# Moving 20 on-chip buffers to other addresses and taking out one small write on GpSimd

## The reference

```python
# attention: B=2, H=8 heads, S=768, D=64, 16 clusters a head
q_assign = argmax(q_n @ c_n.T); k_assign = argmax(k_n @ c_n.T)
mask   = q_assign[..., :, None] == k_assign[..., None, :]
scores = where(mask, scale * q @ k.T, -1e9)
x      = softmax(scores) @ v                      # -> (1536, 512)
# mixture of 8 experts, each row goes to one
e      = argmax(x @ w_gate);  gate = softmax(x @ w_gate)[e]
x      = gate * (relu(x @ w1[e]) @ w2[e])         # w1: 512x1024, w2: 1024x512
# last layer, hidden width 1536
out    = ((x @ w_a) * (x @ w_b)) @ w_out
```

## Time and profile before

| | before |
|---|---|
| median of 3 runs | 809.38 us |
| lowest, highest | 809.35, 809.58 us |
| the profiled execution's own time | 809.58 us |
| its span in the trace | 807.8 us |
| PE busy | 797.6 us (99%) |
| PEld busy | 678.3 us (84%) |
| DVE busy | 459.1 us (57%) |
| ACT busy | 359.0 us (44%) |
| POOL busy | 365.2 us (45%) |

### The profile page before, as it was taken

The page is one execution under the profiler, slowest core; times in us unless marked ns, Lnnn a source line. Parts: engine busy times, 40 slices in busy tenths (PEclk is TensorE's granted clock), DMA queues, the critical chain, the costliest instruction groups (busy, mean ns, idle before and its releaser), DMA issues.

```text
span 807.8 us, 13176 instructions
## 1 busy us (share of the span) xinstructions
PE 797.6 (99%) x4412; PEld 678.3 (84%) x4413; DVE 459.1 (57%) x716; ACT 359.0 (44%) x740; POOL 365.2 (45%) x311
## 2 busy tenths in 40 slices
PE   8999999999999999999999999999999999999997
PEld 5899999999998688888888888888888888888886
DVE  5987988988997989999867004531211112121211
ACT  7877867877786443443434444111212112121112
POOL 6798898888982354464454634000311002010001
PEclk9999999999999999999999999999999999999999
DMA  7463363363242487888677313300101000010001
GB/s 202 115 190 95 105 185 94 102 187 95 63 125 84 152 255 201 250 251 253 220 212 235 113 41 99 123 1 14 27 14 53 1 14 13 1 53 0 1 1 52
DMA packets 48665, 86.62 MB, mean 107 GB/s; under 512 B 17856, under 2 KB 19904, under 8 KB 48624
## 3 DMA queue, kind: packets, MB, share of 16 engines
q1 hardware_dynamic: 41888, 69.36, 29.9%
q0 software_dynamic: 3856, 11.33, 4.9%
q10 hardware_dynamic: 2880, 5.39, 1.8%
HBM read 73.29 MB, written 11.30 MB: 105 GB/s over the span
## 4 chain that ended last, share of the span: by engine, by line
PE 77%; issue 16%; DVE 2%; DMA 2%; POOL 1%; ACT 1%; SPq 0%; POOLq 0%; DVEq 0%
PE bank L1729 9%; PE bank L1659 9%; PE bank L1463 7%; PE bank L1626 7%; PE bank L1628 7%; PE bank L1627 7%; PE bank L1666 4%; PE bank L1733 4%; PE bank L1432 4%; PE bank L1477 4%; PE bank L1453 4%; PE bank L1479 3%; PE bank L1501 2%; PE bank L1391 2%; PE bank L1673 2%
## 5 line engine op out<-in xcount | busy, mean ns | idle before, releaser
L1355 DVE TENSOR_TENSOR ab_raw<-bank,a_sb 128x512 f32<-128x512 f32 x35 | 24.2, 692 | 183.9 <-PE bank L1628 183.9
L409 DVE CAST w_split<-stage 128x1024 fp32r<-128x1024 f32 x68 | 70.0, 1029 | 68.2 <-PE bank L1666 52.7
L1128 DVE TENSOR_REDUCE neg_max<-bank 128x1 f32<-128x768 f32 x96 | 91.6, 955 | 23.4 <-PE bank L1453 22.5
L846 ACT ACTIVATE pT_hi<-bank 128x384 fp32r<-128x384 f32 x192 | 83.9, 490 | 43.0 <-PE bank L1463 42.4
L413 DVE TENSOR_TENSOR w_split<-stage,w_split 128x1024 fp32r<-128x1024 f32 x72 | 99.3, 1382 | 2.4
L1096 DVE TENSOR_TENSOR pT_lo<-bank,pT_hi 128x384 fp32r<-128x384 f32 x192 | 97.5, 550 | 2.2 <-ACT pT_hi L846 1.7
L717 POOL TENSOR_TENSOR hT_lo<-hT_raw,hT_hi 128x512 fp32r<-128x512 f32 x38 | 54.6, 1437 | 78.0 <-ACT hT_raw L921 77.9
L866 ACT ACTIVATE probs<-bank,neg_max 128x768 f32<-128x768 f32 x96 | 87.1, 907 | 3.4 <-DVE neg_max L1128 3.2
L1729 PE MATMUL bank<-w_split,hT_hi 128*128 (+1 forms) x304 | 79.5, 404 | 0.0
L981 ACT ACTIVATE a_sb<-bank 128x512 f32<-128x512 f32 x35 | 20.9, 597 | 131.9 <-PE bank L1628 131.9
L1463 PE MATMUL bank<-ident,probs 128*128 128x128 f32 x576 | 78.9, 273 | 0.1
(11 more groups left out here) (269 smaller groups left out, 1735.9 us busy)
## 6 DMA issues: line engine op xcount, KB each, us to landing
stage<-w SPq DMA_DIRECT2D x64, 512.0 KB, 4.5
q_raw<-qT SPq DMA_DIRECT2D x32, 192.0 KB, 3.7
k_raw<-kT SPq DMA_DIRECT2D x32, 192.0 KB, 4.0
sorted_y<-y_sb ACTq DMA_DIRECT2D x19, 257.0 KB, 4.7
q_pair<-qT SPq DMA_DIRECT2D x8, 384.0 KB, 4.7
v_raw<-v_keys SPq DMA_DIRECT2D x16, 192.0 KB, 4.1
stage<-w_a SPq DMA_DIRECT2D x6, 512.0 KB, 4.6
stage<-w_b SPq DMA_DIRECT2D x6, 512.0 KB, 4.9
```

The costliest lines, as they stand in the source:

```text
L1128: dve.tensor_reduce(neg_max[:, qt % 2:qt % 2 + 1], scores[qt % 2][:, 0:S], AX_X, ALU.max, negate=True).then_inc(s_max, 1)
```

## The change

Two things change, in one edit. First, buffers are declared in another order, and three fillers change in size: `gap_to_x_in` (480 bytes) goes, `last_scope_room` shrinks by 480 bytes, `past_attention` by 3,392. Nothing else about the buffers changes, neither shape nor type. Second, the write at L704 goes, and with it the second increment of `s_spare_i`.

```diff
--- before.py
+++ after.py
@@ -61,16 +61,16 @@
             return ctx.enter_context(nc.semaphore(name))
 
 
-        tri = sb("tri", [P, P], BF16)
-        token_tile = sb("token_tile", [P, T, 1], F32)
         ident = sb("ident", [P, P], F32)
         ident_bf = sb("ident_bf", [P, P], BF16)
         factors = sb("factors", [P, 2], F32)
+        tri = sb("tri", [P, P], BF16)
         ones = sb("ones", [P, P], BF16)
         e_minus = sb("e_minus", [P, T, E], F32)
         row_no = sb("row_no", [P, 1, P], BF16)
         row_no1 = sb("row_no1", [P, 1, P], BF16)
         tile_row = sb("tile_row", [P, 1, TILES], F32)
+        token_tile = sb("token_tile", [P, T, 1], F32)
         token_lane = sb("token_lane", [P, 1], F32)
         slot_row = sb("slot_row", [P, T], I32)
         slot_tile = sb("slot_tile", [P, T], F32)
@@ -100,6 +100,7 @@
         e_start_i = sb("e_start_i", [P, E], I32)
         first_pair = sb("first_pair", [P, T, 2], BF16)
         e_zero = sb("e_zero", [P, T // 2], BF16)
+        spare_i = sb("spare_i", [P, 1], I32)
         first_f = sb("first_f", [P, 1], F32)
         first_i = sb("first_i", [P, 1], I32)
         gate2 = sb("gate2", [P, T], F32)
@@ -122,9 +123,15 @@
 
         att = ExitStack()
         sb("first_expert_weights", [P, HELD, 2, CH], F32R, att)
+        c_minus = sb("c_minus", [P, C], F32, att)
         cen_rows = sb("cen_rows", [P, 2, D], F32, att)
+        exp_spare = sb("exp_spare", [P, 1], F32, att)
+        cen_sq = sb("cen_sq", [P, D], F32, att)
+        cen_n = sb("cen_n", [P, 8], F32, att)
         cen_pair = sb("cen_pair", [P, PAIRS, 2, C], F32, att)
+        mask_line = sb("mask_line", [P, 2], F32, att)
         back_w = sb("back_w", [P, G, XW], F32, att)
+        gate_w = sb("gate_w", [P, H, E], F32, att)
         q_pair = sb("q_pair", [P, S], F32, att)
         k_pair = sb("k_pair", [P, S], F32, att)
         q_raw = sb("q_raw", [P, 2, S], F32, att)
@@ -138,11 +145,6 @@
         hot_rows = sb("hot_rows", [P, S], F32, att)
         probs = sb("probs", [P, 2, S], F32, att)
         o_T = sb("o_T", [P, HALF], F32, att)
-        c_minus = sb("c_minus", [P, C], F32, att)
-        cen_sq = sb("cen_sq", [P, D], F32, att)
-        cen_n = sb("cen_n", [P, 8], F32, att)
-        mask_line = sb("mask_line", [P, 2], F32, att)
-        gate_w = sb("gate_w", [P, H, E], F32, att)
         x_head = sb("x_head", [P, 2, QT, XW], F32, att)
         neg_max = sb("neg_max", [P, 2], F32, att)
         row_sum = sb("row_sum", [P, 2, QT, 2], F32, att)
@@ -155,7 +157,6 @@
         one_hot = sb("one_hot", [P, 2 + 4 * QT, 2 * C], BF16, att)
         pT_hi = sb("pT_hi", [P, 2, QT, HALF], F32R, att)
         pT_lo = sb("pT_lo", [P, 2, QT, HALF], F32R, att)
-        exp_spare = sb("exp_spare", [P, 1], F32, att)
         att.close()
 
 
@@ -167,7 +168,6 @@
         hT_lo = sb("hT_lo", [P, F], F32R, tiles_scope)
         hT_raw = sb("hT_raw", [P, F], F32, tiles_scope)
         y_sb = sb("y_sb", [P, 2, ROW], F32, tiles_scope)
-        sb("gap_to_x_in", [P, 120], F32, tiles_scope)
         x_in = sb("x_in", [P, 2, DM], F32, tiles_scope)
         tiles_scope.close()
 
@@ -178,7 +178,7 @@
         a_sb = sb("a_sb", [P, 512], F32, last_scope)
         ab_raw = sb("ab_raw", [P, 512], F32, last_scope)
         last_scope.close()
-        sb("last_scope_room", [P, 2 * CH * 2 + 2 * DM + 2 * 512 + 128], F32, moe)
+        sb("last_scope_room", [P, 2 * CH * 2 + 2 * DM + 2 * 512 + 8], F32, moe)
 
         turns_scope = ExitStack()
         xT_hi = sb("xT_hi", [P, 2, DM], F32R, turns_scope)
@@ -189,6 +189,7 @@
         abT_hi = sb("abT_hi", [P, 2, 512], F32R, moe)
         abT_lo = sb("abT_lo", [P, 2, 512], F32R, moe)
         sb("after_xT", [P, DM], F32, moe)
+        x2 = sb("x2", [P, 2, ROW], F32, moe)
         x2T_raw = sb("x2T_raw", [P, DM], F32, moe)
 
         routing = ExitStack()
@@ -196,14 +197,12 @@
         row_hot = sb("row_hot", [P, T, P], BF16, routing)
         tile_hot = sb("tile_hot", [P, T, TILES], BF16, routing)
         tile_tokens = sb("tile_tokens", [P, T, 2, TILES], BF16, routing)
-        sb("past_attention", [P, 1808], F32, routing)
+        sb("past_attention", [P, 960], F32, routing)
         lane_hot = sb("lane_hot", [P, T, P], BF16, routing)
         spare_rows = sb("spare_rows", [P, D], F32, routing)
-        spare_i = sb("spare_i", [P, 1], I32, routing)
         routing.close()
 
         x2T_a = sb("x2T_a", [P, 2, DK, 4 * P], F32R, moe)
-        x2 = sb("x2", [P, 2, ROW], F32, moe)
         moe.close()
 
 
@@ -701,7 +700,6 @@
             pool.wait_ge(s_spare, 16)
             pool.wait_ge(s_rows[0], 16 * PAIRS)
             pool.wait_ge(s_rows[1], 16 * (PAIRS + 1))
-            pool.memset(spare_i[:, :], 0).then_inc(s_spare_i, 1)
             pool.wait_ge(s_first, 1)
             gather_x(0, 0)
```

## The result

| | before | after |
|---|---|---|
| median, same chip | 809.44 us | 816.2 us |
| lowest, highest | 809.35, 809.58 us | 815.82, 816.24 us |
| the profiled execution's own time | 809.58 us | 815.69 us |
| its span | 807.8 us | 813.9 us |

The change makes the kernel slower: ratio after to before 1.0083, interval 1.0064 to 1.01. Forecast were 809.1 us and a range up to 810.3; the loss of 6.8 us lies outside it and on the other side.

A forecast was written before the change was run, and what follows sets the result against it. TensorE was taken to bound the kernel, full from 269 to 800 us; the gather's 0.25 us gain, with addresses at 0, took the median from 809.38 to 809.13, rounded 809.1 us, range 808.3 to 810.3.

The forecast's parts named there:

- The addresses, for the engines: Moved operand starts on TensorE, ScalarE, VectorE and GpSimd: claimed no change in time, 0 for each.
- 0.2 ns a matmul for what is unmeasured: Range allowance for unmeasured TensorE reads over 2,099 matmuls: 0.4 us, taken as a further 0.5 us each side.
- slower: operands that straddle: Experts and last layer: operands 32 past a multiple of 64 touch 33 lines instead of 32; 14 us, 823; chance 0.08.
- The write at L704: GpSimd ahead of the first gather: without the write the gather begins 0.32 us sooner, range -0.32 to +0.1.
- The first gather of the earlier trace: Nearest row for the write step: a gather VectorE alone releases, beginning at 272.02, 0.27 us after token_i is ready.
- faster in attention: Attention operands touch 16 lines of 128 bytes instead of 17; 14 us, 795; chance 0.10, with other alignment gains above 1.6 us.
- the other engines' speed on moved buffers: ScalarE and VectorE pay nothing for starts at an odd multiple of 32, GpSimd taken likewise: 0.
- the helpers' cover: GpSimd has 3.53 us free in each pair of heads and must lose all of it before TensorE waits.
- the absence of an effect of the DMAs' addresses: Moved DMA addresses, with the start's k_raw and the x_in gather on the path: 0, within 0.3 us either way.
- an estimate of up to 0.37 us less: Gather of x_in: 8 pieces a row instead of 9, if the 256-byte read rule held for writes; not counted.
- a shift at the first gather goes on to the end: Behind the first gather TensorE is full, so a shift there, taken as 0.25 us, reaches the program's end.
- full to 800 us: TensorE in experts and last layer is busy throughout, waiting by name once from 269 to 800 us, for 0.3 us.

The follow-up runs named there:

- all_32_down: Kernel before with first_f folded into factors, so every large buffer lies 32 bytes lower and distances stay; 809.47 us, ratio 0.9998.
- write_out: Kernel before with only the write at L704 taken out, every address as before; 809.91 us against 809.68, ratio 1.0003.
- mended_256: Kernel after with two larger fillers, putting xT and abT 256 bytes off the weights and x2T_a at a multiple of 256; 810.44 us, ratio 1.0012.
- addresses_only: Kernel after with the write at L704 put back, its addresses kept; 815.76 us, ratio 1.0075.
- the small kernel: Separate kernel of matmuls alone, without the reference's computation, moving the stationary operand's start from line to line; 231.9 us for all of it.
- waits_turned: Kernel before without the write at L704 and with the wait for first_i moved ahead of GpSimd's other waits there; 809.64 us, ratio 1.0002.

## Why the prediction was wrong

**Failed: "The addresses, for the engines", TensorE, "I take 0".** This step looked at where each operand starts and never at where two operands of one matmul start relative to each other. Distances of a multiple of 256 became 32 and 64, and the price was 5.9 us (1.92 in the experts, 3.94 in the last layer). The rows that I bounded it by could not show it. L1501 reads 72 columns, and where 256 or 384 columns were at a distance (32 or 128), they show no effect of it. In before all pairs of large operands in fp32r have distance 0, so no row of its trace held the other case. The trace gave one hint: 226 ns for fp32r against 216 for bf16 was read as a sign that reads in fp32r cost something, which no run has separated from other causes; and I gave 0.2 ns a matmul for what is unmeasured, where those at a distance took 4 to 6 more.

**The rival "slower: operands that straddle"** had the sign, not the cause and not the size. Its operands are those that do straddle in all_32_down, at no cost; it foresaw 14 us evenly over all products, and got 5.9 on those at a distance.

**Failed in sign, small: "The write at L704".** Forecast 0.32 us sooner; measured 0.21 later (write_out, 0.80 against 0.59 behind `first_i`). The step credited the write with time that is there without it: the 0.58 us behind the write were the rest of 0.75 us behind the separate wait ahead of it. The text had the right mechanism as its upper end, "if the waits regroup into one more waiting instruction ... up to 0.1 us is added", and priced it too low: the waiting instruction costs 0.04, but 0.73 us follow it before the gather begins, and it now holds the late condition. The first gather of the earlier trace rows was the wrong neighbour, as no separate wait stands ahead of it.

**Right:** the attention (a pair of heads is 30.7 us both times, so the rival "faster in attention" is out), the other engines' speed on moved buffers, the helpers' cover (no third wait of TensorE), the absence of an effect of the DMAs' addresses that can be told (mended_256 has them moved and lies 0.95 us above before in all; the gather of `x_in`, for which the prediction had an estimate of up to 0.37 us less, took 3.32 us in after and 3.38 in addresses_only, at remainder 0, and 3.35 in before and 3.39 in write_out, at 192), and that a shift at the first gather goes on to the end. The step "full to 800 us" was right too and is why it came out this way: with TensorE full, each ns a matmul reaches the end undiminished.

A page's rule bears on this. The runs: with nothing else at work, the same fp32r matmul is spaced 226.6 or 233 ns by the distance of its two operands alone. The Trainium skill (SBUF — State Buffer, "Who interferes with whom") says that TensorE never waits on anyone. Among engines, no run here contradicts it; within TensorE the runs show a cost of how its two operands lie to each other, of which the sentence doesn't speak. The Trainium skill's formula for the gap of a single matmul at the full clock (TensorE: Matmul & The Clock Gate, "Back-to-back issue gap") gives, as an estimate, 512 / 2.4 + 2.5 = 216 ns; the bf16 lines, though they follow each other, agree with 215.8, the fp32r ones do not, by 11 or by 17 ns.

**Open.** What in the chip makes the distance count was not settled; the runs measure the dependence and no more. Open too is why 192 costs less than 64, 128 and 224, why its spacings repeat in threes, and why `xT_lo` at 16 costs 2.3 ns in the kernel (230.8 against 228.5) where the small kernel shows 6.6.

## What to carry to other kernels

When a full TensorE runs fp32r matmuls of 512 columns, add up the start of both operands of every product and keep their difference a multiple of 256 bytes (0, 256 and 512 were measured by themselves); a reordered buffer or a changed filler anywhere ahead of one of them can cost nearly 3% of each such matmul (6 of 227 ns) without a single wait in the profile. The sign in the trace is fewer matmuls in a stretch where the engine is as full as before; the mean of one line by shape, or eight in a row in the chain, then names the product. A statement taken out of a list of waits also changes which instruction carries which wait, so look for the late condition and see which instruction holds it. Here it cost 0.2 us when a separate wait held it instead of the gather.

## What the runs showed of the hardware that I had not expected

- Spacing of fp32r matmuls of 512 columns: 226.6 ns at a distance of 0, 256 or 512 bytes, 232 to 234 at most others, with little effect of the common start (226.6 to 227.8 with both moved by 32 to 256). bf16 of the same size: 215.8 at 0, 32 and 128. The distance is that of the stationary operand from the moving one, and its sign counts: 228.9 at 192, 233 at 64.
- 16 bytes below a multiple of 256 is cheaper than 16 above: 226.7 at 240 and 228.3 at 496, against 233.2 at 16; in the kernel 228.5 at -16 against 230.8 at 16. At 8 bytes it is the other way: 233 at 504, 230.7 at 8.
- GpSimd began the first gather 0.72 to 0.76 us after the end of the last separate waiting instruction ahead of it, with a write in between (before, 0.75) or without (after, write_out, 0.73), and so 0.55 us behind `first_i` where that wait had ended 0.17 us earlier (waits_turned).
